# One element-wise subtraction per unit goes from VectorE's queue to GpSimd's queue in an fp32 attention, MLP and expert kernel

## The reference

```
kv  = einsum('bhsd,bhse->bhde', k, v);  o = einsum('bhsd,bhde->bhse', q, kv)
x   = rms_norm(o) * g_norm             # 2304 tokens x 512
h   = x @ w_in                         # 512 -> 2048
x2  = (max(h,0) + alpha*min(h,0)) @ w_out
P   = exp(x2 @ w_gate - max), 8 rounds of row and column scaling   # 2304 x 8
out = sum_e P[:, e] * (max(x2 @ w1[e], 0) @ w2[e])                  # 8 experts, 512 -> 1024 -> 512
```

## Time and profile before

| | us |
|---|---|
| median of three runs | 2096.7 (2095.61 to 2097.36) |
| the profiled execution | 2096.7 |
| its span in the trace | 2094.8 |
| period of a plain MLP unit (units 2 to 6) | 17.51 to 17.53 |
| period of a plain expert unit | 15.64 |
| period of the boundaries 7, 15, 23 | 26.57, 26.55, 26.57 |
| period of the boundaries 55, 87 | 19.16 each |

### The profile page before, as it was taken

One profiled execution on the slowest core, in us unless ns is written; L12 is line 12 of the kernel. 1 busy time (PEld: TensorE's weight loads), 2 busy tenths in 40 slices (PEclk: granted clock), 3 DMA queues, 4 the chain that ended last, 5 costly groups with the idle time before them and its releaser, 6 DMA issues.

```text
span 2094.8 us, 25714 instructions
## 1 busy us (share of the span) xinstructions
PE 2003.7 (96%) x10204; PEld 1792.0 (86%) x10204; DVE 1133.1 (54%) x1532; ACT 830.9 (40%) x1390; POOL 917.6 (44%) x739
## 2 busy tenths in 40 slices
PE   7889899899899999999999999999999999999999
PEld 6778687688798988888888888888888888888888
DVE  4756756756748544445464445444455544444543
ACT  5633333333343343433443343443443344343342
POOL 3234434434444454454445444444444445445441
PEclk9999899999999999999999999999999999999999
DMA  9412111112112222212222211222222222222221
GB/s 231 112 41 61 41 60 60 41 60 61 50 52 73 69 61 71 70 61 75 67 86 65 81 61 61 81 61 61 80 61 91 70 72 61 73 69 61 77 65 41
DMA packets 174983, 146.41 MB, mean 70 GB/s; under 512 B 9728, under 2 KB 141840, under 8 KB 174864
## 3 DMA queue, kind: packets, MB, share of 16 engines
q1 hardware_dynamic: 174144, 144.74, 23.2%
q10 hardware_dynamic: 720, 0.03, 0.0%
HBM read 140.01 MB, written 4.72 MB: 69 GB/s over the span
## 4 chain that ended last, share of the span: by engine, by line
PE 84%; DVE 11%; ACT 2%; issue 2%; DMA 0%; ACTq 0%
PE ps L904 14%; PE ps L903 14%; PE ps L902 14%; PE ps L879 13%; PE ps L881 13%; PE ps L882 12%; DVE cb L621 2%; DVE xc L611 2%; DVE w2l L645 2%; DVE neg L618 2%; DVE cb L637 1%; ACT hh L479 1%; PE ps L803 1%; PE ps L813 1%; DVE hh L629 1%
## 5 line engine op out<-in xcount | busy, mean ns | idle before, releaser
L879 PE MATMUL ps<-xc,w1h 128*128 128x384 f32 x1680 | 571.9, 340 | 66.7 <-DVE cb L621 37.8
L904 PE MATMUL ps<-w2h,hh 128*128 128x512 f32 x1440 | 574.5, 399 | 0.0
L371 POOL TENSOR_TENSOR w1l<-raw,w1h 128x768 fp32r<-128x768 f32 x120 | 222.4, 1853 | 803.1 <-ACT w1h L460 803.1
L903 PE MATMUL ps<-w2l,hh 128*128 128x512 f32 x1440 | 571.8, 397 | 0.0
L881 PE MATMUL ps<-xc,w1h 128*128 128x384 f32 x1680 | 569.9, 339 | 0.0
L882 PE MATMUL ps<-xc,w1l 128*128 128x384 f32 x1680 | 565.9, 337 | 0.0
L902 PE MATMUL ps<-w2h,hh 128*128 128x512 f32 x1440 | 563.8, 392 | 0.0
L879 PEld LDWEIGHTS ps<-xc,w1h 128*128 128x128 f32 x1680 | 318.7, 190 | 111.3 <-DVE cb L621 34.5
L375 POOL TENSOR_TENSOR w1l<-tt,w1h 128x1024 fp32r<-128x1024 f32 x120 | 292.3, 2436 | 256.4 <-ACT w1h L466 256.3
L485 ACT ACTIVATE hh<-cb 128x384 fp32r<-128x384 f32 x288 | 151.2, 525 | 508.7 <-DVE cb L637 508.6
L881 PEld LDWEIGHTS ps<-xc,w1h 128*128 128x128 f32 x1680 | 318.9, 190 | 32.5
(11 more groups left out here) (95 smaller groups left out, 1640.2 us busy)
## 6 DMA issues: line engine op xcount, KB each, us to landing
raw<-in_moe_w SPq DMA_DIRECT2D x384, 256.0 KB, 3.4
raw<-in_moe_w_in SPq DMA_DIRECT2D x48, 256.0 KB, 3.9
raw<-in_moe_w_out SPq DMA_DIRECT2D x48, 256.0 KB, 3.0
qkv<-in_q SPq DMA_DIRECT2D x16, 288.0 KB, 7.2
qkv<-in_k SPq DMA_DIRECT2D x16, 288.0 KB, 6.8
qkv<-in_v SPq DMA_DIRECT2D x16, 288.0 KB, 8.6
out<-acc SPq DMA_DIRECT2D x12, 192.0 KB, 2.6
out<-acc SPq DMA_DIRECT2D x12, 128.0 KB, 2.4
```

Of the source, the lines that this page charges most:

```text
L371: nc.gpsimd.tensor_tensor(w1l[:, u % 2, B22:T1, :].rearrange("p m c -> p (m c)"), r[:, KW:4 * KW], w1h[:, u % 2, B22:T1, :].rearrange("p m ...
L879: nc.tensor.matmul(bank, wh, xh, start=i in (M1, M2, M5) and kt == 0, stop=False, skip_group_check=True)
L903: nc.tensor.matmul(ps[:, t, :], hi, wl, start=False, stop=False)
L904: last = nc.tensor.matmul(ps[:, t, :], lo, wh, start=False, stop=closes_sum(u) and i == 1)
```

## The change

Line 645, the subtraction that makes `w2l` for units 1 to 119, is taken out of DVE's queue, where it stood behind the low part of C22. It is put into POOL's queue, behind the two low parts `w1l` of the next unit. Its operands, its shape and its two semaphores stay as they were. The function that does it was there on POOL already (line 380) and the DVE one is deleted.

```
@@ gpsimd
             for u in range(1, UNITS):
                 if u + 1 < UNITS:
                     differences(u + 1)
                     first_low(u + 1)
+                second_low(u)
@@ vector
-            def second_low(u):
-
-                dve.wait_ge(w2_hi, u + 1)
-                nc.vector.tensor_tensor(w2l[:, u % 2].rearrange("p i d -> p (i d)"),
-                                        raw2[:, u % 2].rearrange("p i d -> p (i d)"),
-                                        w2h[:, u % 2].rearrange("p i d -> p (i d)").bitcast(F32),
-                                        ALU.subtract).then_inc(w2_lo, 1)
@@ vector, step(u)
                     block_sum(u, 1, C22, M7, chain_bank(u), m5s[:, :], 3)
                     hidden_low(u, 1, C22)
-                    if u >= 1:
-                        second_low(u)
                 take_sum(u, 2)
```

## The result

| | before | after |
|---|---|---|
| median of four runs, us | 2097.01 (2095.61 to 2097.36) | 2111.15 (2109.38 to 2112.18) |
| span of the profiled execution, us | 2094.8 | 2110.5 |
| plain MLP unit | 17.51 | 17.71; 18.33 to 18.36 in units 6, 12, 20 |
| boundaries 7, 15, 23 | 26.57, 26.55, 26.57 | 27.71, 27.71, 27.72 |
| boundaries 55, 87 | 19.16 | 20.28, 20.31 |

The change makes the kernel slower: the ratio is 1.0067, with an interval of 1.005 to 1.0086, or 14.1 us between the medians. 2109.9 was forecast. One execution of all those behind this document was slow, of the kernel with the memsets: 3924.64 us where the other three took 2065.25 to 2066.52; its ratio leaves it out. Lines of the changed kernel on ACT and DVE are one higher than before (618 is now 619), those of TensorE nine lower, those of POOL the same.

What follows compares the result with a forecast made beforehand. DVE's order from M7 to the last activation was taken to bound MLP units 1 to 23 and the boundaries. Terms 5.6 + 2.6 + 3.6 + 1.6 - 0.2 = 13.2 us on 2096.7 gave 2109.9, range 2100 to 2122.

Steps and rivals of the forecast that it cites:

- The bound: Only MLP units 1 to 23 and the boundaries can move the time; expert units stay at 15.64 us.
- The exclusion: A POOL instruction and a DVE instruction with all tensor operands in SBUF exclude each other; DVE's neg ends 0.21 us behind POOL.
- The price on POOL: The w2l subtraction takes 2.40 us on POOL, with bounds 2.36 and 2.41.
- The plain unit: MLP units 2 to 6, 10 to 14, 18 to 22: each loses 1.65 - 1.69 + 0.41 = 0.37 us, 5.6 in all.
- Units 8, 16, 24: In 8 and 16 the accumulator copy a transpose waits on comes 0.34 us later; 0 for unit 24.
- the boundaries: w2l takes a turn between DVE's steps: 1.20 us late each at 7, 15, 23 and 0.8 each at 55, 87.
- Units 9 and 17: C22 late, less w2l's slot, plus a collision: 1.63 - 1.14 + 0.42 = 0.91 us each.
- The sum: All terms over the whole kernel: 13.2 us on 2096.7, giving 2109.9 us.
- Faster through early turns for DVE: At neg and line 621 of C22, DVE gets in during w2l: about 34 us faster, 2063; chance 0.15.
- The clock giving time back at the boundaries: Shorter second pause keeps TensorE's clock up: 7.2 us back, 2102.7 alone, 2096.5 with line 366 behind 621; chance 0.1.
- POOL keeping its turn: POOL goes from w2l straight to line 361: 0.3 us more per plain unit, 0.7 per boundary, about 2118; chance 0.13.

Runs made afterwards that it cites:

- the kernel with the memsets: The change with w2l filled with zeros by two GpSimd memsets in place of the subtraction from unit 2 on (leaves out work): 2065.95 us, ratio 0.9848 to the kernel before.
- the two runs that split the change: Against the kernel before, the subtraction on GpSimd only in the expert units: 2098.17 us; only in the MLP units: 2110.46 us.
- the run with eight columns: The change with only 8 of the 1,024 columns of w2l computed on GpSimd from unit 2 on (leaves out work): 2059.22 us, ratio 0.9817 to the kernel before.
- The kernel that is the same as before in the MLP: Against the kernel before, the subtraction on GpSimd only in the 96 expert units, on VectorE in the MLP: 2098.17 us, ratio 1.0001.
- the early copy: Against the kernel before, only ACT's copy w2h moved forward from unit 2 on, subtraction in its old place on VectorE: 2101.45 us, ratio 1.0016.
- the two halves: The change with the GpSimd subtraction cut into two instructions of 512 elements a partition: 2107.15 us, ratio 1.0044 to the kernel before.
- the MLP part alone: Against the kernel before, the subtraction on GpSimd only in units 0 to 23, on VectorE in the expert units: 2110.46 us, ratio 1.0063.
- one and a half times the instruction: The change with GpSimd computing the first half of w2l twice, 512 columns and then all 1,024: 2149.31 us, ratio 1.0247 to the kernel before.
- the early place in the MLP: Against the kernel before, ACT's copy and VectorE's subtraction moved forward only in MLP units 2 to 6, 8 to 14, 16 to 22: 2069.65 us, ratio 0.9866.

## Why the prediction was right, point by point

**The bound.** Expert units at 15.64 in both kernels, the loss in the MLP and at boundaries: shown by the two runs that split the change (2098.17 and 2110.46).

**The exclusion.** Shown by the run with eight columns (`w2l` no longer holds `neg`, 52 us less than the change), by the memsets (POOL busy in the same place without reading, 45 us less) and in the rows: the ends are 0.21 behind POOL's end for `neg`, as read from the earlier trace rows. So these two engines meet at more than their semaphores, unlike what is said at the start. Too wide was only "an instruction of POOL": a memset did not hold the two-input instruction.

**The price on POOL.** 2.40 forecast, 2.397 the median of 120. The estimate of 2.25 from the figure of the Trainium skill (GPSIMD Engine Reference, section 3.1) was the worse one.

**The plain unit.** 0.37 forecast, 0.20 measured where the clock stayed up. The order of all meetings was as written. Mis-sized was the start of `w2l`: I put it in the place of line 361, 0.14 us behind the end of line 375, but it was taken up 0.04 before that end (158.68 against 158.72), and all behind it is 0.19 earlier. In the kernel's text line 361 stands behind a wait for the semaphore that line 375 itself sets (`t_lo`), `w2l` only behind one for ACT's copy, which was long there; that this wait is the 0.14 us is read from the queue, not tested.

**The clock.** Here a step was missing. I looked for its effect only at the boundaries. The pause before M2 grew from 1.58 to 1.79 us. Twelve of the 15 plain units have a pause of that length (1.78 to 1.84), and in three of them the clock fell behind it:

```profile
203.15 0.44 PE L870 MATMUL ps<-xc,w1h 128*128 128x384 f32 x1 [1.79 <-DVE cb L622]
...
203.97 0.33 PE L872 MATMUL ps<-xc,w1h 128*128 128x384 f32 x1
204.14 0.47 PE L873 MATMUL ps<-xc,w1l 128*128 128x384 f32 x1
204.41 0.63 PE L893 MATMUL ps<-w2h,hh 128*128 128x512 f32 x1
```

These are TensorE's rows behind the pause of the unit whose period is 18.36; in the unit before (M2 at 185.44, a pause of 1.81) the same matmuls take 0.33 and 0.39. The windows (granted clock third from the end) have 0.66 for the stretch with the fall:

```profile
203.00:208.00 5.00, 4.85 (x17) 4.28 (x18) 3.41 (x5) 2.13 (x4) 1.82 (x1) 0.66 0.01 3
208.00:221.90 13.90, 13.05 (x65) 11.42 (x64) 7.27 (x11) 4.38 (x8) 8.55 (x6) 1.00 0.25 75
```

That these longer pauses are the cause is shown as far as this: with 1.58 to 1.60 us it happened in no plain unit of three kernels, with 1.77 to 1.84 in three units of each of three kernels, with 2.22 to 2.36 in nine units of one. The extra 0.63 us in each of three units (1.9 in all) makes up for most of the 2.6 by which 15 plain units were over-sized. That the row of the plain units came out at 4.9 for 5.6 is luck to that extent.

**Units 8, 16, 24.** 0.34, 0.34 and 0 forecast, -0.31, 2.81 and 1.09 measured. The term of 0.34 was too small. The accumulator copy of unit 8, on which the transpose waits, started 4.41 us behind the sum of C22 before (260.33 and 255.92) and 5.25 behind it in the change, so it came 0.84 later; in unit 16 it was 0.83. ACT's copy of `w2h` is late in these units, so `w2l` was taken up only as `neg` was, and held it for its whole length:

```profile
259.80 2.39 POOL L382 TENSOR_TENSOR w2l<-raw,w2h 128x1024 fp32r<-128x1024 f32 x1 [1.88 <-ACT w2h L472]
259.82 2.58 DVE L619 TENSOR_SCALAR neg<-cb,alphaT 128x384 f32<-128x384 f32 x1
...
264.48 1.28 DVE L651 COPY acc<-ps 128x512 f32<-128x512 f32 x2
```

The rest of these differences goes with the clock. Unit 8 began at the lower level (0.50) in both kernels, for 4.8 us before and for 2.3 in the change. In unit 16 the granted clock was 0.83 on the average (0.91 before), with two falls: one behind the boundary, and one behind a pause of 1.73 us for the accumulator copy (0.94 before). No run tests these units by themselves, and they differ by 0.9 to 1.6 us between executions of the same code (see above).

**Units 9 and 17** (0.91 forecast, 0.95) and **the boundaries** (1.20 and 0.8; 1.15 and 0.76) came as worked out. At 55 and 87 the clock fell too, behind a first pause that had grown from 1.16 to 2.81 us; it did not show in the sum, as the pauses of 1.01 and 1.47 us that followed before were gone or down to 0.28.

**The sum.** 2109.9 was forecast and 2111.15 measured, and this is closer than the terms are. Between the profiled executions the difference is 15.7 us, not 13.2. About 1.9 us from falls of the clock in plain units, 1.1 from unit 24 and 1.4 from the time ahead of unit 1 were in no term, units 8 and 16 were 1.8 too low together, and 0.37 for 0.20 made the plain units 2.6 too high. The mechanism was right; that the number is so near is in part luck.

**The rivals.** Faster through early turns for DVE: `neg` was held for the whole instruction in the change, so no. The clock giving time back at the boundaries: it fell there all the same, with second pauses of 2.58, 2.95 and 3.02 us instead of 3.13, 3.15 and 3.17, and it gave some back in unit 8 only. The kernel that is the same as before in the MLP had 2.96, 2.54 and 3.13, so the length of this pause changes between executions. POOL keeping its turn: `neg` went between `w2l` and line 361, so no.

**Open.** Why the clock falls behind some pauses of 1.8 us and not behind others of the same length in the same place: no run here separates that.

## What to carry to other kernels

An engine with spare time is no free place for work if it shuts another engine out while it works. Ask what the other engine starts in those microseconds, and put the long instruction where that engine idles. Here both the engine and the moment counted. VectorE's own 1.2 us, moved from a stretch where all wait for it to one where nobody does, gave 27.6 us (in the MLP alone), and moving the work to GpSimd at the worst moment cost 14.1. With the early copy in all units, the subtraction in VectorE's idle stretch gave 2073.3 us, and the same work on GpSimd at about that time 2099.2, no gain: GpSimd needs 2.4 us for what VectorE does in 1.2, and shuts VectorE's instructions of that sort out for all of them. And follow a held instruction through the queues behind it: in one run the delay came back through ACT to the very place that had been cleared.

## What the runs showed of the hardware that was not expected

- Pauses of TensorE of 1.77 to 1.84 us before M2 were followed by the lower clock (1.2 GHz) in 3 of the 11 or 12 plain units that had one, at 0.6 to 0.8 us each, and that in each of three kernels (the change, the two halves, the MLP part alone); pauses of 1.44 to 1.60 in no plain unit. With one and a half times the instruction the pause was 2.22 to 2.36 us, and it was 9 of 15, at 0.86 us each. In another place a shorter one was enough: in unit 56 or 88 of three kernels (the memsets, the early copy, the early place in the MLP) the clock fell behind a pause of 1.45 to 1.47 us that followed other, mostly shorter pauses of the boundary ahead of it, and such a unit took 18.1 instead of 16.5; in the kernel before, pauses of the same lengths there were followed by no fall.
- The clock did not fall at once: in unit 6 the matmuls became slower at 204.14, 1.0 us after TensorE had started again at 203.15, and in unit 12, where it had started again at 328.97, the granted clock was 1.00 till about 330.5 and 0.50 behind that.
- A memset of POOL's holds the one-input `neg` (0.58 us instead of 0.42) but not a two-input instruction of DVE's (0.56 under it); a subtraction of POOL's holds both.
- At a meeting of two such instructions the one taken up first went first, and here 0.03 us decided it (161.75 against 161.78), so such collisions can't be planned to the tenth of a microsecond.
